# Fused linear attention, mixture of experts and token mixing on one core: the last batch's first z and output split moved ahead, and the first mixed tile summed within the next fold

## The reference

```python
theta = x @ w_theta
zr, zi = x * np.cos(theta), x * np.sin(theta)
y = einsum('ts,bsd->btd', w_tok_r, zr) + einsum('ts,bsd->btd', w_tok_i, zi)
u = x + y
out = u + np.maximum(u @ w_ch, 0.0)
```

## Time and profile before

| | before |
|---|---|
| runs, us | 578.1, 578.65, 581.05 |
| median, us | 578.65 |
| profiled execution, us | 577.51 |
| its span, first to last instruction, us | 575.8 |
| granted TensorE clock | 1.00 of full |
| TensorE busy | 541.0 us, 94% |
| VectorE busy | 372.1 us, 65% |
| ScalarE busy | 298.5 us, 52% |
| GpSimd busy | 131.6 us, 23% |

### The profile page before, as it was taken

How to read it: one execution, slowest core, us unless ns; L and a number is a source line. 1 busy time by engine, 2 the same in 40 slices (tenths; PEclk the granted TensorE clock), 3 DMA queues, 4 the chain that set the end, 5 groups by cost and what they waited for, 6 DMA issues and landing times.

```text
span 575.8 us, 14106 instructions
## 1 busy us (share of the span) xinstructions
PE 541.0 (94%) x5996; PEld 508.3 (88%) x5996; DVE 372.1 (65%) x672; ACT 298.5 (52%) x599; POOL 131.6 (23%) x88
## 2 busy tenths in 40 slices
PE   0989998999999999999999899999999999999997
PEld 0789877998889997899977799999999999999997
DVE  2987888778888687865767677455236544463424
ACT  5668687665867648733578564324232433133311
POOL 2013045045510035100123157112211212022100
PEclk9999999999999999999999999999999999999999
DMA  8938012062210530003500000010001100010002
GB/s 286 346 120 302 2 34 79 3 243 76 69 30 2 177 128 2 2 2 123 210 1 2 1 1 1 1 56 28 1 1 42 41 1 1 14 69 2 1 1 82
DMA packets 17969, 37.24 MB, mean 65 GB/s; under 512 B 2160, under 2 KB 10608, under 8 KB 17392
## 3 DMA queue, kind: packets, MB, share of 16 engines
q1 hardware_dynamic: 17904, 36.32, 18.3%
HBM read 31.46 MB, written 4.72 MB: 63 GB/s over the span
## 4 chain that ended last, share of the span: by engine, by line
PE 77%; DVE 10%; ACT 7%; issue 3%; DMA 2%; SPq 1%; DVEq 0%; ACTq 0%
PE bank L1213 18%; PE bank L1214 18%; PE bank L1215 18%; ACT prob L718 5%; PE bank L1355 4%; PE bank L1418 3%; PE bank L1231 3%; PE bank L1316 3%; PE bank L1276 3%; PE bank L1312 2%; DMA OT<-w_theta 2%; PE bank L1513 1%; PE bank L1297 1%; ACT probT L759 1%; PE bank L1261 1%
## 5 line engine op out<-in xcount | busy, mean ns | idle before, releaser
L1213 PE MATMUL bank<-z_h,wt_h 128*128 128x384 f32 x288 | 97.7, 339 | 1.5 <-DVE z_l L936 1.5
L1214 PE MATMUL bank<-z_l,wt_h 128*128 128x384 f32 x288 | 97.4, 338 | 0.0
L1215 PE MATMUL bank<-z_h,wt_l 128*128 128x384 f32 x288 | 96.5, 335 | 0.0
L718 ACT ACTIVATE prob<-bank,nmax 128x384 f32<-128x384 f32 (+5 forms) x96 | 60.2, 637 | 20.2 <-DVE nmax L1095 20.2
L520 POOL TENSOR_TENSOR trig<-trig,x 128x768 f32<-128x768 f32 x18 | 33.6, 1864 | 152.0 <-ACT trig L630 92.6
L1095 DVE TENSOR_REDUCE nmax<-bank 128x1 f32<-128x384 f32 (+5 forms) x96 | 54.9, 617 | 9.9 <-PE bank L1361 5.2
L951 DVE TENSOR_SCALAR turns<-bank 128x384 int32<-128x384 f32 x22 | 12.2, 556 | 72.9 <-PE bank L1215 72.9
L1213 PEld LDWEIGHTS bank<-z_h,wt_h 128*128 128x128 f32 x288 | 54.0, 188 | 2.2 <-issue 1.9
L1214 PEld LDWEIGHTS bank<-z_l,wt_h 128*128 128x128 f32 x288 | 54.1, 188 | 0.0
L1215 PEld LDWEIGHTS bank<-z_h,wt_l 128*128 128x128 f32 x288 | 54.0, 188 | 0.0
L827 ACT CAST uT_h<-bank 128x384 fp32r<-128x384 f32 x24 | 11.5, 478 | 81.0 <-PE bank L1513 81.0
(11 more groups left out here) (177 smaller groups left out, 1400.1 us busy)
## 6 DMA issues: line engine op xcount, KB each, us to landing
V<-v SPq DMA_DIRECT2D x4, 1152.0 KB, 10.6
gate<-fT SPq DMA_DIRECT2D x12, 384.0 KB, 3.2
q<-qT SPq DMA_DIRECT2D x12, 384.0 KB, 5.8
k<-kT SPq DMA_DIRECT2D x12, 384.0 KB, 6.3
wt_raw<-w_tok SPq DMA_DIRECT2D x6, 768.0 KB, 8.4
out<-x SPq DMA_DIRECT2D x24, 192.0 KB, 1.9
gate<-fT SPq DMA_DIRECT2D x3, 512.0 KB, 5.1
q<-qT SPq DMA_DIRECT2D x3, 512.0 KB, 9.8
```

The costliest lines, as they stand in the source:

```text
L718: nc.scalar.activation(prob[:, m % 2, r, at], bank[r][:, at], ACT.Exp, bias=nmax[:, m, k:k + 1], accum_out=den[:, m // 2, which, e:e + 1]) ...
L1213: nc.tensor.matmul(o, a_h, b_h, start=start, stop=False)
L1214: nc.tensor.matmul(o, a_h, b_l, start=False, stop=False)
L1215: return nc.tensor.matmul(o, a_l, b_h, start=False, stop=stop)
```

## The change

In ScalarE's loop over j of the last batch, token weight 4 moves from j = 5 to j = 6, behind `z_hi(0, 0)` and `copy_turned(5)`, and `split_outputs(0)` follows it there instead of standing at j = 7 behind `copy_portion(2)`. In VectorE's loop `split_outputs(0)` moves ahead of `weigh_outputs(2)` at j = 7. In the last stage, `fold` is cut in two: `fold_first` (L951, L953) stays ahead of `add_x(0)`, `fold_rest` (L956, L959) follows it, in batches 0 to 2. All other folds keep their order. No instruction is added or removed.

```diff
                         if j < 1:
                             token_weights(0)
-                        elif 2 <= j < 2 * TOKENS_FIRST:
+                        elif 2 <= j < JOBS - 1:
                             token_weights(j - 1)
-                        if j == JOBS + 1:
+                        elif j == JOBS:
+                            token_weights(JOBS - 2)
                             split_outputs(0)
-                            token_weights(2 * TOKENS_FIRST - 1)
+                        elif j == JOBS + 1:
+                            token_weights(JOBS - 1)
...
-            def fold(b, s):
+            def fold_first(b, s):
...
                                                op0=ALU.mult, op1=ALU.add).then_inc(r1_done, 1)
+
+            def fold_rest(b, s):
+
+                rs, whole = r_of(b, s), turns_of(b, s)
                 dve.wait_ge(r1_done, upto(b, NT, s + 1))
...
+            def fold(b, s):
+
+                fold_first(b, s)
+                fold_rest(b, s)
...
+                    if it > B - 2 and j == JOBS + 1:
+                        split_outputs(0)
                     if j >= 3 and j % 2 == 1:
                         weigh_outputs((j - 3) // 2)
-                    if it > B - 2 and j == JOBS + 1:
-                        split_outputs(0)
...
                 if it < B - 1:
-                    fold(it + 1, 0)
+                    fold_first(it + 1, 0)
                 add_x(0)
+                if it < B - 1:
+                    fold_rest(it + 1, 0)
```

## The result

The changed kernel takes 573.27 us (median of 4 runs, 572.97 to 573.49) against 578.42 us before (4 runs, 578.1 to 581.05). The ratio is 0.9906, with a 95% interval of 0.9888 to 0.9923. The forecast was 574.2, within 572.7 to 576.9.

A forecast was written before the change was run, and what follows sets the result against it. TensorE, busy in 94% of the span, was taken to bound the kernel; closing its gaps gives 1.61 + 0.55 + 2.25 = 4.4 us off the 578.65 us median, so 574.2 us, range 572.7 to 576.9.

The forecast's parts named there:

- the five named: TensorE's waits from 322 us: three on the first add (1.8 us), z's half (1.54), the split output (0.39); 3.7 us.
- Z first: Last batch: z ahead of the token weight on ScalarE lets the first mixing matmul start sooner; gain 1.61 us.
- The split: Last batch: output's split moved up on ScalarE and VectorE removes the wait ahead of the output product; gain 0.55 us.
- The turns: Last mixing step, three batches: first add within the fold lets TensorE turn the tile without waiting; 0.75 us each, 2.25 together.
- the overlap of the first matmuls: Reason for the range's lower end, 1.5 us under the forecast: this overlap gives another 0.3 us.
- Z's length: VectorE's half of z takes 0.95 us instead of 2.01, as its twin row does with GpSimd idle.
- Rival 1: GpSimd's weight blocks spread on VectorE, whose margin is 0.15 us; gain only 3.6 us, time 575.0; chance 0.13.
- the price of the other order: If spread comes second to GpSimd's weight, the copy of probabilities ends 0.7 to 0.8 us after TensorE wants it.
- Rival 2: Only one part pays, for instance TensorE's gap moves from first to second tile; 2.2 us left, 576.4; chance 0.11.
- Rival 4: Slower: GpSimd running at the three turns stretches the fold's rest, making the second add late; 582.6 us; chance 0.03.

The follow-up runs named there:

- e1: Kernel before with only the last batch's reordering (token weight behind z, both halves of the split moved up), fold undivided: 576.66 us, ratio 0.9961.
- e2: Kernel before with only the fold divided around the first add, last batch's loops as before: 576.01 us, ratio 0.9955.
- e3: Kernel before with only the token weight moved behind z and the copy on ScalarE; split and fold as before: 577.22 us, ratio 0.9972.
- e5: Kernel before with only the output's split moved up on ScalarE and VectorE; token weight and fold as before: 577.67 us, ratio 0.9990.
- e9: Changed kernel with the first add ahead of the whole fold: 576.72 us, ratio 0.9969.
- e10: Changed kernel with the fold divided in batch 0 only, whole and ahead of the add in batches 1 and 2: 576.25 us, ratio 0.9939.
- e11: Changed kernel with GpSimd's half of the value weights in batch 0 waiting for VectorE's four clamps of batch 1: 572.76 us, ratio 0.9893.
- the repeat: The changed kernel run once more, unaltered, beside the kernel before on the same chip: 573.84 us, ratio 0.9911.
- e4: Kernel before with one added wait: GpSimd's token weight for the fifth tile waits until z's low half is written: 577.29 us, ratio 0.9981.
- e6: Changed kernel with ScalarE's token weight straight behind z, ahead of the copy of turned probabilities: 573.90 us, ratio 0.9905.

## Why the prediction was right

**The bound and the places.** TensorE from 322 us on ran without a gap but for the five named, each gap disappeared when its cause was moved, and none came in its place. Taking the edits one at a time (e1, e2, e3, e5) gave sums that add to within 0.05 us, which is what a single saturated engine looks like.

**The terms.** Z first: 1.61 forecast, 1.61 measured between the marks of the weighting and the mixing, of which 0.03 were given back before the next weighting. The split: 0.55 and 0.55. The turns: 0.75 each forecast, 0.82 measured. The missing 0.07 is for the most part the matmul behind the turn, which follows by 0.24 us when the turn did not wait (369.33 to 369.57) and by 0.30 when it did; I had named the overlap of the first matmuls among the reasons for the range and left it out of the sum. Together 4.41 forecast and 4.59 measured. Had I counted idle time alone, it would have been 3.7.

**The median** moved by 5.15 us, half a microsecond more than the trace of the changed stretch explains, and stands 0.9 us under the forecast. Of that, 0.2 us is the median before (578.42 here, 578.65 where the forecast started), 0.2 us the terms above, and the rest is that half microsecond, which the prediction did not foresee. The profiled executions differ by only 4.12 us, because the one before reached the first mark 0.49 us earlier. The uncertain part is the head: the same kernel before ran from 577.49 to 582.19 over later runs. The traces of e9, e10 and e11 show one cause of such scatter. Whether it favours the changed kernel or only this set of runs is open; the repeat gave 0.9911. So the traces confirm the mechanism and its terms; the half microsecond, which no term explains, moved the median away from 574.2 and not towards it.

**What was half right.** Z's length: the cause was GpSimd, as the rows of the same shape suggested, and e4 shows it. Rival 1: spread did come first, by 0.2 us (0.15 forecast); the price of the other order was put at 0.7 to 0.8 us and not measured by itself, since in e4 and e6 TensorE was also late for another reason. What the held portions added between mixing and weighting there was 0.25 us in e4 and 0.05 us in e6. The split's half took 2.40 us where I had 1.75, inside the 1 us that I had granted it. Rival 2 was real as a danger: e9 shows the gap moving to the second tile. Rival 4 was not run; GpSimd was idle at all three turns (its next starts, at 378.20, 440.04 and 501.88, follow 17.4, 19.8 and 19.8 us of idleness).

## What to carry to other kernels

Size a gap by the distance between starts, beside the same pair of instructions where nothing waits: here that gave 4.4 of 4.6 us, idle time 3.7. When a split is made by two engines in turn, move both halves or neither, and check what then stands behind the second. An instruction that looks twice as long as its twin is worth a look at the other engine's timeline: holding GpSimd back by one wait won 0.8 us in e4, with no work removed.

## What the runs showed of the hardware

- GpSimd and VectorE held each other up in these rows, each time until the other's instruction was nearly or wholly done, and where the starts lie 0.1 us or more apart it is the second that was held. Second, z's half took 2.01 instead of 0.95 us, spread 2.17 instead of 0.69, and GpSimd's own weight 2.18 instead of 1.82. What I had not expected is that an instruction of VectorE with one tensor as input and 8 elements per partition waits as long as a large one (share, 1.81 instead of 0.16 us in e6), and so do the clamps (2.27 instead of 0.61 us in e10). VectorE's copy out of a bank was not held: beside GpSimd's weight (323.21 in the changed kernel) it took 1.08 us, as it did before with GpSimd idle. The Trainium skill (SBUF — State Buffer, Who interferes with whom) says that a tensor_scalar can enter a mode in which it takes the shared port pair, that the other engine then "fully blocks", and that issue order decides; by that rule, the trace agrees.
- GpSimd started 0.56 us after the first clamp in e10 and 0.71 us after it in the changed kernel. With these 0.15 us goes a difference of 2.9 us at the first mark: a clamp held up, ScalarE's copy behind it, 1.2 us more idle time on TensorE, and a granted clock of 0.57 from 48 to 52 us. In e1, with the same clamp held up and 1.6 us of waiting, the clock did not fall.
